# The experts' up product as seven block products in place of eight

## What is computed

```
x: [1152, 512]   w1: [4, 512, 1024]   w2: [4, 1024, 512]
p = domain_probs / (domain_probs.sum(-1, keepdims=True) + 1e-09)
for e in range(4):
    h = np.maximum(x @ w1[e], 0.0)
    out += p[:, e:e + 1] * (h @ w2[e])
```

## Time and profile before

| what | value |
|---|---|
| median of three runs | 655.79 us (655.76 to 655.83) |
| the profiled execution, its own time | 655.72 us |
| its span in the profile | 653.9 us |
| outside the span | 1.8 us |
| PE busy | 644.4 us, 99% of the span, 3688 matmuls |
| PEld busy | 600.6 us, 92% |
| DVE, ACT, POOL busy | 289.0, 232.1, 91.2 us |
| TensorE clock granted | full in every slice |

### The profile page before, as it was taken

The page is one execution under the profiler, slowest core; times in us unless marked ns, Lnnn a source line. Parts: engine busy times, 40 slices in busy tenths (PEclk is TensorE's granted clock), DMA queues, the critical chain, the costliest instruction groups (busy, mean ns, idle before and its releaser), DMA issues.

```text
span 653.9 us, 9966 instructions
## 1 busy us (share of the span) xinstructions
PE 644.4 (99%) x3688; PEld 600.6 (92%) x3688; DVE 289.0 (44%) x708; ACT 232.1 (35%) x583; POOL 91.2 (14%) x87
## 2 busy tenths in 40 slices
PE   8999999999999999999999999999999999999998
PEld 7789999999999999999898989898989898989896
DVE  5986764677556575512242412242412252512121
ACT  5887665565445563401131301131301040402020
POOL 1453333233333332000000000000000000000000
PEclk9999999999999999999999999999999999999999
DMA  8914220132000020200030300030400030110101
GB/s 331 352 47 175 75 121 2 33 130 96 1 2 1 33 97 33 98 0 1 0 128 1 130 0 1 0 128 0 128 0 0 0 128 0 64 49 0 48 0 48
DMA packets 11569, 40.56 MB, mean 62 GB/s; under 512 B 2320, under 2 KB 2320, under 8 KB 10256
## 3 DMA queue, kind: packets, MB, share of 16 engines
q1 hardware_dynamic: 11536, 40.13, 17.0%
HBM read 37.77 MB, written 2.36 MB: 61 GB/s over the span
## 4 chain that ended last, share of the span: by engine, by line
PE 95%; DMA 1%; DVE 1%; POOL 1%; ACT 1%; issue 0%; SPq 0%; DVEq 0%
PE ps L720 25%; PE ps L755 20%; PE ps_pT L720 10%; PE ps_score L720 10%; PE ps_score L755 10%; PE ps L740 8%; PE ps_score L740 4%; PE ps_o L740 4%; PE ps_score L681 2%; DMA raw_b<-in_w_out 1%; PE ps_pT L707 1%; PE ps_pT L694 1%; PE ps L762 1%; ACT prob L353 1%; DVE prob L496 0%
## 5 line engine op out<-in xcount | busy, mean ns | idle before, releaser
L442 ACT ACTIVATE hid_hi<-ps 128x384 fp32r<-128x384 f32 x48 | 23.6, 492 | 241.6 <-PE ps L720 241.6
L720 PE MATMUL ps<-xy_hi,wa_hi 128*128 128x384 f32 (+1 forms) x320 | 109.1, 341 | 0.0
L720 PE MATMUL ps<-xy_hi,wa_lo 128*128 128x384 f32 (+1 forms) x320 | 107.3, 335 | 0.0
L720 PE MATMUL ps<-xy_lo,wa_hi 128*128 128x384 f32 (+1 forms) x320 | 107.1, 335 | 0.0
L306 POOL TENSOR_TENSOR sp_c<-sp_e,sp_c 128x384 f32<-128x384 f32 x48 | 64.5, 1344 | 134.7 <-DVE sp_c L512 134.7
L755 PE MATMUL ps<-wb_hi,hid_lo 128*128 128x512 f32 x192 | 74.9, 390 | 0.0
L755 PE MATMUL ps<-wb_lo,hid_hi 128*128 128x512 f32 x192 | 74.9, 390 | 0.0
L755 PE MATMUL ps<-wb_hi,hid_hi 128*128 128x512 f32 x192 | 74.7, 389 | 0.0
L660 DVE SCALAR_TENSOR_TENSOR part<-ps,gate,part 128x512 f32<-128x512 f32 x24 | 18.0, 751 | 104.8 <-PE ps L755 104.8
L720 PEld LDWEIGHTS ps<-xy_hi,wa_hi 128*128 128x128 f32 x320 | 60.1, 188 | 1.4
L720 PEld LDWEIGHTS ps<-xy_lo,wa_hi 128*128 128x128 f32 x320 | 60.1, 188 | 0.4
(11 more groups left out here) (115 smaller groups left out, 1247.5 us busy)
## 6 DMA issues: line engine op xcount, KB each, us to landing
unit_in<-in_units SPq DMA_DIRECT2D x8, 1024.0 KB, 7.0
raw_a<-in_w SPq DMA_DIRECT2D x16, 512.0 KB, 4.2
raw_b<-in_w SPq DMA_DIRECT2D x16, 512.0 KB, 3.8
raw_a<-in_w_in SPq DMA_DIRECT2D x8, 512.0 KB, 5.3
raw_b<-in_w_out SPq DMA_DIRECT2D x8, 512.0 KB, 4.0
out_dram<-part SPq DMA_DIRECT2D x9, 256.0 KB, 2.0
part<-in_units SPq DMA_DIRECT2D x2, 1024.0 KB, 12.3
unit_in<-in_units SPq DMA_DIRECT2D x2, 384.0 KB, 6.5
```

What stands on the lines that cost most here:

```text
L442: act.activation(hid[0][:, f, :], up_banks[f % 4][:, 0:CH], ACT.Relu).then_inc(h_hi, 1)
L720: m = pe.matmul(bank[:, 0:CH], wa[a][:, f, k, :], xy[x][:, bass.ds(c, 1), k, :], start=(k == 0 and i == 0), stop=(k == KT - 1 and i == 2))
```

## The change

The experts are done in 8 pairs q (`PAIRS`): expert q // 2, and one half of its 1024 hidden columns (w1's piece is 512 x 512). In a pair the up product is treated as a 2 by 2 product of blocks. A is w1's piece in four blocks of 256 x 256 (`A11`, `A12`, `A21`, `A22`), B is the MLP's output in four blocks of 256 features by 576 tokens (`B11`, `B21` and, for the other half of the tokens, blocks of which `B22` is used as it is). The product is formed from seven block products of sums of blocks in place of eight of the blocks (Strassen's scheme in Winograd's form). The sums of A (`asum`, four of them, 128x256 elements for each half i of the pair's hidden columns) are formed by DVE in `a_sums`; all seven operands of A are rounded by ACT (`a_high`) and get their low parts on DVE (`a_low`). The sums of B (`T1` to `T4`) are formed once, by DVE, and serve all pairs.

A product `product(q, p, i)` is 12 matmuls of 288 columns: two column blocks s in two banks, two contraction tiles k, three terms. With seven products and two halves i a pair has 168 of them where the kernel before has 144 of 384 columns for the same work (its 1152 in all become 1344). `Z` and `Y` are pairs of PSUM banks: P1, P6, P7 and P4 accumulate in `Z[i]`, one on top of another, P2 starts `Y[i]`, and P5 with P3 fill it again. Between them ACT copies a state of the banks to SBUF (`keep_first`, `keep_second`, `keep_fifth`) and DVE adds a bank to such a copy (`add_c11`, `add_c22`, `add_c12`), all 576 elements wide. `relu_high` and `relu_low` work on 576 elements from these sums, for the blocks C11, C22, C21 and C12. `down_tokens(q, T)` then does nine tiles of 128 tokens with 12 matmuls of 512 columns each (864 in all as before), and `add_tokens` adds each to `acc`.

Also changed: `y_high`, `y_low` and `clear_sums` go; their place takes `b_high` (ACT) and `b_low` (DVE), fifteen rounds over pieces of B and T, in the steps 35 to 44 and at the start of the experts; every buffer has a fixed address; the experts' loops are unrolled on all engines; w1 is laid out on the host so that a piece holds four blocks.

The diff, cut to its core ("..." marks what is left out):

```diff
-        def sb(name, shape, dt=F32):
...
+        def sb(name, offset, shape, dt=F32):
+            return nc.alloc_sbuf_tensor_at(name, shape, dt, offset=BASE + offset)
...
+        PLACES = {"B11": (0, 18432), "B21": (4608, 23040), "T2": (9216, 27648), "T1": (13824, 32256),
+                  "T3": (92160, 96768), "T4": (101376, 105984), "B22": (110592, 115200)}
+        bop = {name: [sb(f"{name}_hi", at[0], [P, 2, HALF], F32R), sb(f"{name}_lo", at[1], [P, 2, HALF], F32R)]
...
+        Z = [bank_pair[0][:, :, 0:HC], bank_pair[2][:, :, 0:HC]]
+        Y = [bank_pair[1][:, :, 0:HC], bank_pair[3][:, :, 0:HC]]
...
+        CAST_AFTER_SUMS = {1: 13, 2: 14, 3: 15, 4: 16, 5: 18, 6: 20, 10: 20, 15: SUMS}
+        CAST_AFTER_TSUM = {7: 2, 8: 1, 9: 3, 11: 5, 12: 4, 13: 6, 14: 8}
+        READY = {"B11": 5, "B21": 6, "T2": 11, "T1": 12, "T3": 13, "T4": 14, "B22": 15}
...
+        PRODUCTS = {"P1": (0, "B11"), "P2": (1, "B21"), "P6": (4, "T2"), "P5": (3, "T1"),
+                    "P7": (5, "T3"), "P4": (2, "T4"), "P3": (6, "B22")}
+        ORDER = [("P1", 0), ("P2", 0), ("P1", 1), ("P2", 1)] + [
+            (p, i) for p in ("P6", "P5", "P7", "P4", "P3") for i in range(2)]
...
+        TOKEN_BANKS = [single[0][0], single[0][1], single[2][0], single[2][1], single[0][0],
+                       single[1][0], single[1][1], single[3][0], single[3][1]]
...
-                sp.wait_ge(down_read, KT * 6 + TT * 3 * (NE - 1) + T + 1)
+            for q in range(PAIRS):
+                for i in range(2):
+                    if q == 0:
+                        sp.wait_ge(wa_hi, 14 + 2 * i)
+                        sp.wait_ge(wa_lo, 14 + 2 * i)
+                    else:
+                        sp.wait_ge(a_lo, 4 * (2 * q - 2 + i) + 4)
+                    sp.dma_start(raw_a[:, i, :, :], w1[q // 2, q % 2, i]).then_inc(raw_a_in[i], 16)
+                for i in range(2):
+                    at = 14 + 2 * i if q == 0 else 16 + 4 * (q - 1) + 2 * i + 2
+                    sp.wait_ge(wb_hi, at)
+                    sp.wait_ge(wb_lo, at)
...
+            def keep_first(q, i):
+                act.wait_ge(prod_done, product_count(q, "P1", i))
+                if q > 0:
+                    act.wait_ge(eh_lo, hidden_count(q - 1, "C12", i))
+                act.activation(kept[i][:, :, :], Z[i], ACT.Copy).then_inc(p1_copied, 1)
+            def keep_second(q, i):
+                act.wait_ge(prod_done, product_count(q, "P6", i))
+                act.wait_ge(eh_lo, hidden_count(q, "C11", i))
+                act.activation(kept[i][:, :, :], Z[i], ACT.Copy).then_inc(u2_copied, 1)
+            def keep_fifth(q, i):
+                act.wait_ge(prod_done, product_count(q, "P5", i))
+                act.activation(fifth[i][:, :, :], Y[i], ACT.Copy).then_inc(p5_copied, 1)
...
+            def relu_high(q, b, i):
+                if b == "C21":
+                    act.wait_ge(prod_done, product_count(q, "P4", i))
+                else:
+                    act.wait_ge({"C11": c11_added, "C22": c22_added, "C12": c12_added}[b], 2 * q + i + 1)
+                act.activation(hidden_place(ehid[0], b, i), hidden_source(b, i), ACT.Relu).then_inc(eh_hi, 1)
...
+            def t_step(place, a, b):
+                dve.tensor_tensor(place, a, b, ALU.subtract).then_inc(t_sum, 1)
...
+            def late_first():
+                dve.wait_ge(down_read, SUMS - 2)
+                t_step(straddling(0), late(yc[:, 2, 0:2, :]), straddling(0))
+            def late_second():
+                dve.wait_ge(down_read, SUMS)
+                dve.wait_ge(t_sum, 4)
+                t_step(late(tsum[:, :, N0:HALF]), late(yc[:, 2, 2:4, :]), straddling(0))
+            def late_third():
+                t_step(yc[:, 2, 0:2, :], yc[:, 2, 2:4, :], yc[:, 2, 0:2, :])
...
+            def a_sums(g):
+                a11, a12, a22, a21 = [raw_u[:, g % 2, i, :, :] for i in range(4)]
+                s1, s2, s3, s4 = [asum[:, i, :, :] for i in range(4)]
+                dve.wait_ge(raw_a_in[g % 2], 64 + 16 * (g // 2 + 1))
+                if g > 0:
+                    dve.wait_ge(a_lo, 4 * g)
+                dve.tensor_tensor(s1, a21, a22, ALU.add).then_inc(a_sum, 1)
+                dve.tensor_tensor(s3, a11, a21, ALU.subtract).then_inc(a_sum, 1)
+                dve.wait_ge(a_sum, 4 * g + 1)
+                dve.tensor_tensor(s2, s1, a11, ALU.subtract).then_inc(a_sum, 1)
+                dve.wait_ge(a_sum, 4 * g + 3)
+                dve.tensor_tensor(s4, a12, s2, ALU.subtract).then_inc(a_sum, 1)
...
+            def add_c11(q, i):
+                dve.wait_ge(prod_done, product_count(q, "P2", i))
+                dve.wait_ge(p1_copied, 2 * q + i + 1)
+                dve.tensor_tensor(kept[i][:, :, :], Y[i], kept[i][:, :, :], ALU.add).then_inc(c11_added, 1)
+            def add_c22(q, i):
+                dve.wait_ge(prod_done, product_count(q, "P7", i))
+                dve.wait_ge(p5_copied, 2 * q + i + 1)
+                dve.tensor_tensor(fifth[i][:, :, :], Z[i], fifth[i][:, :, :], ALU.add).then_inc(c22_added, 1)
...
+            def relu_low(q, b, i):
+                dve.wait_ge(eh_hi, hidden_count(q, b, i))
+                dve.scalar_tensor_tensor(out=hidden_place(ehid[1], b, i), in0=hidden_source(b, i), scalar=0.0,
+                                         in1=f32(hidden_place(ehid[0], b, i)), op0=ALU.max,
+                                         op1=ALU.subtract).then_inc(eh_lo, 1)
...
+            def add_tokens(q, T):
+                e = q // 2
+                dve.wait_ge(tokens_done, N_TOK * q + T + 1)
+                if q == 0:
+                    dve.tensor_scalar(acc[:, T, :], TOKEN_BANKS[T], gate[:, T, e:e + 1], None,
+                                      ALU.mult).then_inc(out_added, 1)
+                else:
...
-            expert(NE - 1, False, True)
+            for i in (7, 8, 9, 10):
+                b_low(i)
+            last = NB1 * NCH - 1
+            first_out(last, 0)
+            first_out(last, 1)
+            first_out(last, 2)
+            late_first()
+            first_out(last, 3)
+            late_second()
+            late_third()
+            b_low(11)
+            b_low(12)
+            for q in range(PAIRS):
+                add_c11(q, 0)
+                add_c11(q, 1)
+                relu_low(q, "C11", 0)
+                relu_low(q, "C11", 1)
+                if q == 0:
+                    b_low(13)
...
+                add_c22(q, 1)
+                relu_low(q, "C22", 0)
+                relu_low(q, "C22", 1)
...
+                relu_low(q, "C21", 0)
+                relu_low(q, "C21", 1)
...
+                    pair_down_low(0, 3)
+                add_c12(q, 0)
+                add_c12(q, 1)
+                relu_low(q, "C12", 0)
+                relu_low(q, "C12", 1)
+                g = 2 * q + 2
+                for T in range(N_TOK):
+                    add_tokens(q, T)
+                    if q + 1 < PAIRS:
+                        if T in (0, 3):
+                            a_sums(g + T // 3)
+                        elif T in (1, 4):
+                            a_low(g + T // 3, 0)
+                            a_low(g + T // 3, 1)
+                        elif T in (2, 5):
+                            a_low(g + T // 3, 2)
+                            a_low(g + T // 3, 3)
...
+            def product(q, p, i):
+                if p == "P1":
+                    pe.wait_ge(a_lo, 4 * (2 * q + i) + 4)
+                if q == 0:
+                    pe.wait_ge(b_lo, READY[PRODUCTS[p][1]])
+                    if p == "P1" and i == 0:
+                        pe.wait_ge(bank_read, STEPS - 2)
+                    elif p == "P2" and i == 0:
+                        pe.wait_ge(bank_read, STEPS)
+                    elif p == "P1":
+                        pe.wait_ge(down_read, SUMS - 2)
+                    elif p == "P2":
+                        pe.wait_ge(down_read, SUMS)
+                elif p == "P1":
+                    pe.wait_ge(out_added, N_TOK * (q - 1) + (5 if i == 0 else 4))
+                elif p == "P2":
+                    pe.wait_ge(out_added, N_TOK * (q - 1) + (7 if i == 0 else 9))
+                if p in ("P6", "P5", "P7", "P4", "P3"):
+                    pe.wait_ge({"P6": p1_copied, "P5": c11_added, "P7": u2_copied,
+                                "P4": c22_added, "P3": p5_copied}[p], 2 * q + i + 1)
+                row, name = PRODUCTS[p]
+                into = (Y if p in ("P2", "P5", "P3") else Z)[i]
+                fresh = p in ("P1", "P2", "P5")
+                for s in range(2):
+                    for k in range(2):
+                        for j, (a, b) in enumerate(TERMS):
+                            m = pe.matmul(into[:, s, :], aop[a][:, i, row, k, :], bop[name][b][:, k, HC * s:HC * s + HC],
+                                          start=(fresh and k == 0 and j == 0), stop=(k == 1 and j == 2),
+                                          skip_group_check=not fresh)
```

(23 more changed lines are left out.)

373 lines of the change are left out of this document (226 added, 147 removed).

## The result

The changed kernel takes 633.27 us (median of four runs, 633.19 to 633.9) beside 655.77 us for the kernel before in the same job. The ratio is 0.966, with a 95% interval of 0.9644 to 0.9677. The forecast was 635.3 us with a range from 633.5 to 640.0 us: the direction came as forecast, but the time lies 2.0 us under the forecast and 0.2 us under the range's low end.

What follows compares the result with a forecast made beforehand. The prediction took PE alone, gapless over the experts, as the bound: 655.72 us less 20.5 us for the exchanged matmuls is 635.2, plus 0.1 us for a tight margin gives 635.3 us, range 633.5 to 640.0 us.

Steps and rivals of the forecast that it cites:

- The bound: Experts: PE alone sets the time, with chunks of 33.02 us and no gap, so fewer columns shorten the kernel.
- Nobody is waited for: Pairs and first pair: DVE and ACT work stays hidden behind PE, costed at nothing; tightest steady slack 0.65 us at P4.
- a brush: First pair: 0.1 us added to the sum in case one of the 0.5 us margins is touched.
- The first: Rival: the first pair stalls on its preparation rows, time 636 to 639.3 us; chance 0.12.
- the second rival: The handover from DVE at P4 fails in every pair, 638.5 us or 641.7 us; chance 0.07.
- The third rival: Every product: weight loads bind and the kernel gets slower, break-even 148.6 ns between loads, up to 708.7 us; chance 0.05.
- The mechanism of the gain: Experts' up products: 1152 matmuls of 384 columns removed, 1344 of 288 added, -20.5 us on PE.
- the price of the matmuls: Up products: 199.7 us removed at 173.3 ns each, 179.2 us added at 133.3 ns each; 512-column matmuls held constant.
- the cheap bound of one term: Price of 288 columns by a straight line through both measured widths: 132.7 ns, gain -21.3 us.
- The fourth rival: Up products: the fixed part of a matmul shrinks with the width, down to 120.0 ns, 617.3 to 633.5 us; chance 0.03.

Runs made afterwards that it cites:

- handover_1: Changed kernel with one more 576-element addition on DVE ahead of each `add_c22`, from the second pair on; 634.64 us.
- w_sweep: Changed kernel with the products of pairs 0 to 7 computing only 288 down to 128 of each 288 columns, output incomplete; 612.12 us.
- p1_twice: Changed kernel with each first product P1 computed twice, so eight products of 288 columns in place of seven; 659.09 us, ratio 1.0051.
- split_304: Changed kernel with a product's 576 columns cut into 304 and 272 in place of 288 and 288; 630.48 us, ratio 0.9618.
- more_waits: Changed kernel with four long-fulfilled waits ahead of each matmul group of the token tiles; 633.45 us.
- order_ksj: Changed kernel with a product's 12 matmuls ordered contraction tile, column block, term; 634.57 us, ratio 0.9684.
- order_kjs: Changed kernel with a product's 12 matmuls ordered contraction tile, term, column block; 634.16 us, ratio 0.9672.
- before_unrolled: Kernel before the change with the loops over experts and chunks written out on all engines; 656.06 us, ratio 1.0001.

## Where the prediction held, and where it failed

**The bound.** The argument from the earlier trace rows that PE alone sets the experts' time, and that there is no gap to fill or to be lost, held to the last piece of the chain.

**Nobody is waited for.** Each handover came in time. P4 of the steady pairs has 0.46 us to spare where the forecast had 0.65 to 0.75, which counted up to the matmul, 0.13 us behind its weight load. In the first pair thirteen rows of preparation stand on DVE ahead of `add_c11`, not the eleven that were counted ahead of the result. Some of them, and what follows, as a timeline:

```profile
256.98 0.96 DVE L727 TENSOR_TENSOR tsum<-part 128x768 f32<-128x768 f32 x1
...
258.86 0.96 DVE L724 TENSOR_TENSOR T_lo<-tsum,T_hi 128x768 fp32r<-128x768 f32 x1
...
267.04 1.36 DVE L724 TENSOR_TENSOR T_lo<-tsum,T_hi 128x1152 fp32r<-128x1152 f32 x1 [1.23 <-ACT T_hi L511]
268.32 0.76 DVE L789 TENSOR_TENSOR fifth<-banks,fifth 128x576 f32<-128x576 f32 x1
...
275.38 1.28 DVE L778 TENSOR_TENSOR wb_lo<-raw_b,wb_hi 128x512 fp32r<-128x512 f32 x2
```

T2's low part ends at 259.82 (forecast 260.3), T4's at 268.40 (269.0), `add_c22` at 269.08 (269.7), C21's last low part, which stands ahead of the row at 275.38, near 275.4 (276.1). All are 0.5 to 0.7 us earlier than worked out; since PE is 0.44 us earlier as well, the margins are those of the forecast within 0.3 us. P6's first matmul has its record at 260.15, 0.33 us after T2's low part (forecast 0.5), and its weight load starts 0.13 us before that. The 0.1 us that I added for a brush with such a margin was not spent, but only 0.15 us were left (260.02 - 259.82 - 0.05). The first and the second rival did not happen; `handover_1` shows how near the second one is: one more row of 0.67 us on DVE begins to cost.

**The loads do not bind.** At 132.7 ns they follow with room; the floor is 111.4 ns (`w_sweep`), where the earlier trace rows gave 110 to 112. The third rival needed 148.6 ns.

**The mechanism of the gain.** One block product in eight is not computed, and PE is the only bound: `p1_twice` puts the product back and loses 25.8 us. That part of the forecast held. What failed are the sizes of its terms, and with them the range.

**The step that failed is the price of the matmuls.** The forecast took "120.0 ns for the columns and the 13.3 ns that the 384 wide ones pay", 133.3 ns, with 132.7 ns as a bound. It is 132.72 ns, 0.8 us less over 1344 matmuls. The second part of the step is a term that was put at nothing, the change from one width to the other. The 384 wide ones were put at 2.08 / 12 = 173.3 ns from a piece of one tile, while a whole chunk of the kernel before (its chain of work, 96 of L720 from 287.40, then 72 of L755) gives more:

```profile
287.40 4.18 PE ps L720 x24
...
295.74 4.16 PE ps L720 x24
...
304.06 10.92 PE ps L755 x48
314.98 5.44 PE ps_score L755 x24
```

(304.06 - 287.40) / 96 = 173.5 ns, 173.6 from the records' starts; and the 72 take 16.36 us, 227.2 ns, not 227.5. The two errors cancelled in the 33.02 us by which I had tested them. And the token tiles were held constant, but cost 226.8 ns after.

The steady prices are 4.16 / 24 = 173.3 ns and 5.44 / 24 = 226.7 ns, before and after the change. The rest stands in the first tile behind each change of width, where a few distances are longer. By the records' starts, the first 24 matmuls of 512 columns of a chunk take 5.48 in place of 5.44 us (12 times, 0.5 us), and the first 12 of 384 columns behind a token tile 2.106 in place of 2.080 us (11 times, 0.3 us). In the changed kernel the first token tile of a pair takes 2.73 in place of 2.72 us (8 times, 0.1 us). So 173.3 ns was the right steady price, and the changeovers are what the sum lacked.

Luck has a part here. The bound of 132.7 ns, which the measurement hit, came from a line through 227.5 ns, which has a changeover in it; through the steady 226.7 ns the line gives 133.3 ns. And the estimate of -22.6 us from the Trainium skill (TensorE: Matmul & The Clock Gate, Back-to-back issue gap) lies close to the whole gain of 22.5 us, though its distances are too short here, 122.5 ns against 132.7 and 162.5 against 173.6. The section calls that formula the gap of an isolated matmul and gives other figures for a stream.

| term | forecast | measured | us |
|---|---|---|---|
| 1344 matmuls added | 133.3 ns | 132.7 ns | -0.8 |
| 1152 matmuls removed | 173.3 ns | 173.6 ns | -0.3 |
| 864 of 512 columns, after against before | 0 | 226.8 against 227.2 ns | -0.4 |
| start of the last `up` of the MLP | 243.99 | 243.55 | -0.4 |
| margin for a brush | 0.1 | 0 | -0.1 |
| sum | | | -2.0 |

The sum is the whole difference between 635.3 and 633.3. What each is caused by is known in unequal degree. That the part beyond the columns isn't a constant is shown: 12.7 ns in the changed kernel, 11.7 with the first 288 columns read twice, 13.2 and 13.3 in the two other orders, 10.6 in the mean of `split_304`. The table's -0.3 and -0.4 us are the changeovers. `more_waits` rules out fulfilled waits as their cause; with the same token tiles the first one of a pair takes 2.72 us in `split_304` and 2.77 us in `order_ksj`, so it hangs on the products ahead of it. What makes it stays open. The start is scatter between runs of the same work (243.26 to 244.22), and the profiled run of the kernel before lay in the upper part.

**The range.** Its low end, 633.5, stood at the cheap bound of one term (-21.3 us in place of -20.5 gives 634.5) and 1 us on top. Three further errors of 0.3 to 0.4 us, each under what I thought worth pricing, had the same sign. The fourth rival (617.3 to 633.5) has the measured time in its upper corner, and was given 0.03. A fixed part that shrinks with the width is what `w_sweep` shows, but at 288 columns it gives 0.6 ns of the rival's 13.3, and `order_kjs` pays 13.2 ns at the same width.

**Chances.** With 3.4% gained, "faster" at 0.92 was right, and by the route that was given for it; the 0.70 for 634.0 to 636.0 us was not.

## What to carry to other kernels

Where TensorE is the only bound, an algorithm with fewer products is worth its share of the matmuls, less what the narrower tiles cost, and was priced here to 0.3% of the time from the distance between starts. Price each kind of matmul from a whole stretch, with the change of width in it, and compare that with a steady piece; and give the sum's small terms a width of their own. Where a matmul waits for another engine, count the spare time up to its weight load and not to the matmul, and take the handover off. Before a tiling is fixed, try neighbouring cuts of the moving tile: 304 and 272 columns instead of twice 288 were worth 3.0 us here, with the same work.

## What the runs showed of the hardware

- A stream of 128 x 128 fp32r weight loads, each with its matmul, doesn't go below 111.4 ns at the full clock: 112.2 ns at 240 columns, 111.4 at 128.
- Above the floor a matmul costs its columns and, in the mean of a product, 10.6 to 14.1 ns more (13.3 at 384 and at 512 columns in a steady stream). This part hangs on which columns are read and how the tile is cut, in steps that no rule of this study orders (130.55 ns at 304, 133.05 at 306). The bank that is written has no part in it.
- Where the width changes from matmul to matmul, the first tile costs up to 0.04 us more in these kernels (5.48 against 5.44 us before, 2.73 against 2.72 after, nothing in `split_304`).
- A matmul's wait holds back its weight load as well: a release that comes at the matmul's time is 0.13 us late for the load, and after such a delay two distances are long (218 and 238 ns), not one.
- A wait that is fulfilled and an unrolled loop cost TensorE nothing that can be measured here (`more_waits`, `before_unrolled`).
- A weight load's busy share of 100% goes with distances from 111 to 126 ns alike.
